# Loading the keys on two DMA queues instead of one: the odd key groups are issued on ScalarE's queue

## The reference, cut to what matters

```
kv_pool = kv.reshape(1, 96, 4, 8, 4, 128).mean(axis=(2, 4))    # 768 pooled keys, each the mean of 16
k = v = kv_pool.reshape(1, 768, 128) @ w_sr
a = softmax(q @ k.T / sqrt(128));  x = a @ v                   # attention, 12288 rows
h = x @ w_in1;  g = 0 if h <= -1, h if h >= 1, else (h+1)**2/4;  y = g @ w_out1
h = y @ w_in2;  g = h * sigmoid(1.702 h);                        out = g @ w_out2
```

## Time and profile before

| | before |
|---|---|
| median of 3 runs | 1296.47 us (1295.76 to 1298.28) |
| the profiled execution | 1296.52 us, of which the span from first to last instruction 1294.7 us |
| TensorE matmuls busy | 1270.7 us, 98% of the span |
| GpSimd busy | 1145.9 us, 89% |
| granted TensorE clock | 1.000 over the span |
| DMA | 35.72 MB in all, 12.71 MB of it in the first 80 us |

### The profile page before, as it was taken

How to read it: one execution, slowest core, us unless ns; L and a number is a source line. 1 busy time by engine, 2 the same in 40 slices (tenths; PEclk the granted TensorE clock), 3 DMA queues, 4 the chain that set the end, 5 groups by cost and what they waited for, 6 DMA issues and landing times.

```text
span 1294.7 us, 17016 instructions
## 1 busy us (share of the span) xinstructions
PE 1270.7 (98%) x5494; PEld 1022.8 (79%) x5494; DVE 991.1 (77%) x1138; ACT 1006.1 (78%) x1070; POOL 1145.9 (89%) x491
## 2 busy tenths in 40 slices
PE   6989999999999999999999999999999999999998
PEld 2656888888888888888888888888888888888876
DVE  5778878878779788787797887877978879776443
ACT  3677787888787878887878788878787888797666
POOL 4828999999999999999999999999999999979780
PEclk9999999999999999999999999999999999999999
DMA  9110000000000000010000000000000000000000
GB/s 347 34 29 9 22 24 21 18 18 33 16 16 21 18 27 16 16 33 16 16 17 19 29 16 16 33 16 17 16 19 30 16 17 25 9 17 17 1 9 17
DMA packets 18258, 35.72 MB, mean 28 GB/s; under 512 B 3248, under 2 KB 3376, under 8 KB 17968
## 3 DMA queue, kind: packets, MB, share of 16 engines
q1 hardware_dynamic: 18224, 35.30, 8.5%
HBM read 28.90 MB, written 6.39 MB: 27 GB/s over the span
## 4 chain that ended last, share of the span: by engine, by line
PE 89%; POOL 5%; issue 3%; DVE 2%; ACT 1%; DMA 0%; POOLq 0%; SPq 0%; ACTq 0%; DVEq 0%
PE ps_ring L505 16%; PE ps_ring L506 16%; PE ps_ring L507 16%; PE ps_y L505 12%; PE ps_y L506 12%; PE ps_y L507 12%; POOL g_lo L411 4%; PE ps_y L661 1%; PE ps_ring L532 1%; PE ps_two L595 0%; DMA q_sb<-in_q_t 0%; POOL pt_lo L411 0%; DVE g L1126 0%; ACT g L909 0%; ACT g L904 0%
## 5 line engine op out<-in xcount | busy, mean ns | idle before, releaser
L411 POOL TENSOR_TENSOR g_lo<-g,g_hi 128x1024 fp32r<-128x1024 f32 x363 | 922.9, 2573 | 74.1 <-DVE g L1126 64.4
L1117 DVE SCALAR_TENSOR_TENSOR g_hi<-g,ps_ring 128x1024 fp32r<-128x1024 f32 x182 | 221.7, 1218 | 144.0 <-ACT g L909 143.9
L890 ACT ACTIVATE g<-ps_ring 128x1024 f32<-128x1024 f32 x192 | 197.2, 1027 | 168.5 <-PE ps_ring L507 168.3
L505 PE MATMUL ps_y<-g_hi,w_hi 128*128 128x512 f32 x748 | 294.5, 394 | 3.5 <-POOL g_lo L411 2.3
L506 PE MATMUL ps_y<-g_lo,w_hi 128*128 128x512 f32 x748 | 291.3, 389 | 0.0
L507 PE MATMUL ps_y<-g_hi,w_lo 128*128 128x512 f32 x748 | 291.2, 389 | 0.0
L1126 DVE SCALAR_TENSOR_TENSOR g<-g,ps_ring 128x1024 f32<-128x1024 f32 x192 | 232.8, 1212 | 8.0 <-ACT g L909 8.0
L909 ACT ACTIVATE g<-g 128x1024 f32<-128x1024 f32 x192 | 204.3, 1064 | 5.4
L904 ACT ACTIVATE g<-ps_ring 128x1024 f32<-128x1024 f32 x192 | 197.9, 1031 | 8.9 <-PE ps_y L661 7.7
L892 ACT ACTIVATE g_hi<-ps_ring 128x1024 fp32r<-128x1024 f32 x192 | 195.9, 1020 | 6.1 <-PE ps_y L507 6.1
L505 PEld LDWEIGHTS ps_y<-g_hi,w_hi 128*128 128x128 f32 x748 | 140.4, 188 | 41.1 <-POOL g_lo L411 9.9
(11 more groups left out here) (135 smaller groups left out, 1681.8 us busy)
## 6 DMA issues: line engine op xcount, KB each, us to landing
kv_sb<-in_kv_t SPq DMA_DIRECT2D x12, 512.0 KB, 9.1
q_sb<-in_q_t SPq DMA_DIRECT2D x24, 256.0 KB, 3.7
out_t<-y_sb SPq DMA_DIRECT2D x24, 256.0 KB, 3.5
key_max<-max_row SPq DMA_DIRECT2D x23, 256.0 KB, 3.4
inv_sum<-inv_row SPq DMA_DIRECT2D x23, 256.0 KB, 3.3
w_raw<-in_moe_w_in SPq DMA_DIRECT2D x2, 1024.0 KB, 17.0
max_row<-max_turned SPq DMA_DIRECT2D x23, 2.0 KB, 1.3
inv_row<-inv_turned SPq DMA_DIRECT2D x23, 2.0 KB, 1.3
```

The source lines that it names most:

```text
L411: return nc.gpsimd.tensor_tensor(dst, src, upper.bitcast(F32), ALU.subtract)
L505: nc.tensor.matmul(dst, l_hi, r_hi, start=start, stop=False)
L890: nc.scalar.activation(g2[:, slot, :], ps_h2(it, k), ACT.Gelu_apprx_sigmoid).then_inc(g2_done, 1)
L1117: nc.vector.scalar_tensor_tensor(out=g1_hi[:, uu % 2, :], in0=g1[:, uu % 2, :], scalar=1.0, in1=ps_h1(it, k), op0=ALU.min, op1=ALU.max).th ...
```

## The change

The odd groups are left out of SyncE's loop and issued at the head of ScalarE's program, all six in a row, ahead of its first copy.

```diff
@@ SyncE
             for g in range(KG):
                 keys = slice(g * GK, (g + 1) * GK)
-                sp.dma_start(kv_sb[:, keys, :], kv_t[:, keys, :]).then_inc(kv_loaded[g], 16)
+                if g % 2 == 0:
+                    sp.dma_start(kv_sb[:, keys, :], kv_t[:, keys, :]).then_inc(kv_loaded[g], 16)
                 if g == 1:
                     sp.dma_start(q_sb[:, 0, :], q_t[:, 0:T]).then_inc(q_loaded[0], 16)
                 if g == 3:
@@ ScalarE
+            for g in range(1, KG, 2):
+                keys = slice(g * GK, (g + 1) * GK)
+                nc.scalar.dma_start(kv_sb[:, keys, :], kv_t[:, keys, :]).then_inc(kv_loaded[g], 16)
             act.wait_ge(w_turned, 1)
             copy(wsr_t[:, :], ps_two[:, 0, 0:C], SCALE / WIN).then_inc(w_scaled, 1)
```

## The result

The changed kernel takes 1301.44 us (median of 14 runs, 1298.62 to 1303.92), the kernel before 1297.49 us in the same job (14 runs, 1295.76 to 1299.69): ratio 1.0032, 95% interval 1.0025 to 1.0039. It is slower by 4 us where 1.3 was forecast, outside the range, and the whole interval lies above the 0.2% that the prediction took as the least that can be told from no change.

What follows compares the result with a forecast made beforehand. TensorE, busy 98% of the span, was taken as the bound, with the change acting only through the start. The sum was 1296.52 + 0 + 0 + 1.3 = 1297.8 us, range 1295.2 to 1300.5.

Steps and rivals of the forecast that it cites:

- What bounds the kernel, and where the change acts: Whole kernel: TensorE is busy 98% of the span, so the change acts only through the start, sliding everything behind it.
- The prediction's own sign of being wrong: Start against end: the prediction is wrong if the end moves by more than the start of line 518 did.
- What the query tile waits for: First query tile's load: odd groups on ScalarE's queue share the full DMA engines and delay it, +1.3 us taken.
- even turns by transfer or by bytes: Queue sharing at the start: one more group ahead of the tile, +1.28 us, or 0.8 us by bytes; chance 0.50.
- rival A: Queue sharing at the start: queues alternate packet by packet, two more groups ahead, +2.6 us, 1299.1 us; chance 0.17.
- the prediction's slope: Loads at the start: 1.28 us per key group of 512 KB, from the landings of groups 6 and 9.
- The rest of the chain slides as a whole: Compute behind the query tile, up to the loop: each piece is released by the one before, so all slides together.
- Rival D: TensorE's ramp: if its rate still rises at about 14 us, half the delay passes, 1297.1 us; chance 0.13.
- Costs put at nothing: Issue time on SyncE and ScalarE, table load, copy to `wsr_t`, later keys and weights: cost 0.
- my half microsecond of cover: Late even groups: group 4's sum ends at 18.2 against 18.7 us needed; group 6 has 0.4 us of cover.

Runs made afterwards that it cites:

- second repeat of the change: The changed kernel run a third time without any edit, for another profile: 1299.38 us in one run.
- first repeat of the kernel before: The kernel before run again without any edit, for another profile: 1296.07 us in one run.
- half-length rows: The changed kernel with each odd group issued as two transfers with 2 KB rows, three groups ahead of the first copy, three behind: 1299.91 us, ratio 1.0018.
- five filled starts: Small unread multiplications before the first projection, some with ten larger ones later; kernel before: ratios 0.9997, 1.0000, 0.9988; changed kernel: 1.0034, 1.0028.
- last version's: The kernel before with seven small multiplications ahead of the projection and ten larger ones ahead of the step waiting for `y_lo`: 1295.37 us, ratio 0.9988.

## Why the prediction was wrong, point by point

**What bounds the kernel, and where the change acts.** Right. The sliding ramp passes to the end undiminished: the difference at the first unit of layer 1 is 4.40 us on average, and the medians are 3.95 apart. For the second repeat of the change against the first repeat of the kernel before it is 3.32 us at the first unit and 3.31 us in the time. The prediction's own sign of being wrong, that the end moves by more than the start of line 518, came true: 4.79 us against 1.69 in the profiled executions.

**What the query tile waits for.** The right term, mis-sized. I took even turns by transfer or by bytes, one group more ahead, +1.28 us. It was rival A, turns by packet, +2.6 us by that rival's count; measured +1.69 in the one profile, +2.07 over three. The count of that rival was right, three whole odd groups by 9.2 us. It came out lower in time because the stream of keys also begins earlier, at ScalarE's issue at 0.73 instead of 1.18: by 6 us the DMA engines had moved 1.48 MB, against 1.29 before, and 0.19 MB is 0.5 us at the prediction's slope. The half-length rows and the query tiles on the other queue separate this from even bytes, and the rows of `w_sr` speak against turns by whole transfer. I had the sizes of the packets in hand and gave the rival that used them 0.17.

**The second query tile** was missing from the sum. I checked the key groups behind the first tile one by one, and skipped the transfer that stands among them: it is delayed twice, once by the odd groups beside tile 0 and once by those beside itself. Its projection waited 0.44, 0.60 and 0.47 us for it in the three profiles, which is the 0.5 beyond the first wait (2.57 less 2.07). It was a term put at nothing without a reason.

**The rest of the chain slides as a whole.** This step cost about as much as the tile's wait. Between the start of tile 1's projection and the last maximum another 1.84 us were lost (4.41 less 2.57), all of it in multiplications that took 2.07 us a pair instead of about 1. A halved rate is what TensorE's lower level would give, 1.2 instead of 2.4 GHz. The clock column of the stretches does not show it, it reads 1.00 in them; but the traces' record of the granted clock only begins with the rise to the full rate, at 14.2 and 13.4 us in two profiles of the kernel before and at 20.6 and 22.8 us in two of the change (the third of each has no such entry), which is where the long products end.

Where the products take the same times, the step holds. The second repeat of the change and the first profile of the kernel before have 1.73 and 1.72 us for the projection of tile 1 and 1.12 and 1.13 for the scores behind it; they differ by 2.72 us at that projection, by 2.75 at the last maximum and at the first unit of layer 1, and by 2.86 in the time. So the two query tiles are worth about 2.7 us, and the rest is the rate.

Rival D saw the clock and had its sign wrong: it let the rise stay at 14 us and the late start gain by it. In these profiles it came later, at 17 to 23 us. Why is open. The time of TensorE's first work alone does not set it: with the queries on the second queue the projection started at 4.39, earlier than in any other run, and the products were slow until about 17.5; with three groups moved it started at 11.39, later than with the change, and they were at full rate from 18.6. That idling is the cause is argued from the five filled starts, where the short gaps went with the full rate; the medians of the filled kernels don't confirm it, except for the last version's.

**A later stretch at half the rate** in the profiled execution of the change explains why that one lost 4.79 us and not 4.1:

```profile
90.00:92.00 2.00, 0.71 (x2) 0.48 (x3) 2.00 (x3) 2.00 (x3) 1.77 (x1) 1.00 0.00 0
92.00:96.00 4.00, 4.00 (x9) 2.31 (x9) 1.51 (x7) 2.33 (x3) 0.00 (x0) 0.57 0.01 2
```

After 2.8 us without a product, up to 91.3 us, the granted clock falls to 0.57 on average (the third number from the end), and the next product of line 662 takes 2.84 us instead of 2.00. The repeats of both kernels show no such stretch, and the kernel before idles for 2.8 us in the same place, up to 87.1 us, without one. It belongs to the execution.

**Costs put at nothing.** Issue time on both engines, the table load, `wsr_t` (at 5.53, forecast 5.3), the weights: nobody waited for them, as forecast. Groups 4 and 6 came 1.5 and 0.5 us later than forecast and stayed hidden only because the scores were late too; my half microsecond of cover would not have held.

## What to carry to other kernels

A transfer on the critical path is delayed by what runs beside it on another queue as well as by what stands ahead of it on its own; when the DMA engines are full, loads that are moved to a second queue can pass it; here they did so packet for packet, and the queue with the short rows lost. Put the transfer that the chain waits for at the head of a queue, and check every transfer behind it against its own consumer. A delay at the start cost up to as much again here in slow multiplications, and their share changed from one execution to the next, so a start is compared over several profiles, and over profiles from both clusters where the times fall in two.

## What the runs showed of the hardware

- Two queues on full DMA engines alternate by packet: 137 to 135 packets with rows of 4 KB against 2 KB, 0.50 to 0.26 MB.
- A DMA issued at 10.6 us on an idle queue, beside a full one, sent its first packet 3.5 us later; issued at 0.73 us it took 1.2 us.
- The same program lands its first query tile between 9.2 and 9.8 us from one execution to another, and runs its multiplications at the lower rate until 17 to 23 us; the kernel before lands it at 7.3 to 7.5 us in three profiles, and with the same order of loads once at 8.8. This makes one profile of each kernel a poor measure of differences of 1 to 2 us.
